# Second weight's sums alone through scratch, its plain blocks split in place, and the second phase's first loads on ScalarE's queue

## The reference, cut to what matters

```python
def reference(q, k, v, U, V, w_ch1, w_ch2, w_in, w_spatial, b_spatial, w_out):
    # windowed attention: batch 4, 8 heads, 576 tokens, head size 64, window 128
    x = attention(q, k, v)                      # (4, 576, 512)
    u = x + (x^T @ U @ V)^T                     # rank 32, over the tokens
    x = u + maximum(u @ w_ch1, 0) @ w_ch2       # w_ch1 512 x 2048, w_ch2 2048 x 512
    h = maximum(x @ w_in, 0); a, g = halves(h)
    g = layernorm(g); g = w_spatial @ g + b_spatial
    return (a * g) @ w_out                      # (4, 576, 512)
```

## Time and profile before

| what | us |
|---|---|
| median of 3 runs | 771.54 |
| lowest and highest | 770.56, 773.52 |
| the profiled execution, device time | 773.02 |
| its span, first to last instruction | 771.2 |
| PE busy in the span | 728.5 |
| VectorE busy | 454.9 |
| ScalarE busy | 339.0 |
| GpSimd busy | 180.3 |

### The profile page before, as it was taken

How to read it: one execution, slowest core, us unless ns; L and a number is a source line. 1 busy time by engine, 2 the same in 40 slices (tenths; PEclk the granted TensorE clock), 3 DMA queues, 4 the chain that set the end, 5 groups by cost and what they waited for, 6 DMA issues and landing times.

```text
span 771.2 us, 13217 instructions
## 1 busy us (share of the span) xinstructions
PE 728.5 (94%) x4688; PEld 671.2 (87%) x4688; DVE 454.9 (59%) x1036; ACT 339.0 (44%) x764; POOL 180.3 (23%) x187
## 2 busy tenths in 40 slices
PE   7999999988999978997679999999999999999998
PEld 5777777778999978997669999999999999998998
DVE  7778777888473247323495895795647417435431
ACT  5977777754352232222134444434343242342422
POOL 1868516410019999200000000000010000100100
PEclk9999999999999988998899999999999999999999
DMA  7689563155448997698975625754680010100101
GB/s 233 224 284 344 185 231 101 61 180 178 151 157 282 315 342 237 238 382 328 414 256 179 212 66 182 233 182 151 239 326 1 25 38 0 46 15 0 61 0 62
DMA packets 82514, 137.68 MB, mean 179 GB/s; under 512 B 5536, under 2 KB 57248, under 8 KB 81568
## 3 DMA queue, kind: packets, MB, share of 16 engines
q1 hardware_dynamic: 82464, 137.03, 51.2%
HBM read 80.06 MB, written 56.95 MB: 178 GB/s over the span
## 4 chain that ended last, share of the span: by engine, by line
PE 68%; DVE 12%; DMA 7%; POOL 5%; issue 4%; ACT 3%; SPq 1%; DVEq 0%; ACTq 0%; POOLq 0%
PE bank L1837 4%; PE bank L1839 4%; PE bank L1838 4%; PE bank L1679 3%; PE wide L1694 3%; PE bank L1876 3%; DMA r_scr<-late 3%; PE bank L1877 3%; PE bank L1878 3%; PE bank L1985 2%; PE bank L1987 2%; PE bank L1986 2%; PE bank L1804 2%; PE bank L1802 2%; PE bank L1803 2%
## 5 line engine op out<-in xcount | busy, mean ns | idle before, releaser
L1837 PE MATMUL bank<-xs,w1s 128*128 128x384 f32 x336 | 115.9, 345 | 9.9 <-DVE tok L1393 8.7
L1839 PE MATMUL bank<-xs,w1s 128*128 128x384 f32 x336 | 114.6, 341 | 0.0
L1838 PE MATMUL bank<-xs,w1s 128*128 128x384 f32 x336 | 114.6, 341 | 0.0
L868 POOL TENSOR_TENSOR vl<-vr,vh 128x512 fp32r<-128x512 f32 x8 | 11.3, 1407 | 401.5 <-ACT vh L1146 401.5
L1022 ACT ACTIVATE rk<-tok 128x768 fp32r<-128x768 f32 x72 | 60.6, 847 | 91.5 <-PE wide L1878 30.4
L1876 PE MATMUL bank<-rk,w2q 128*128 128x384 f32 x208 | 72.1, 347 | 18.4 <-DVE rk L1400 11.2
L1005 ACT ACTIVATE sums_u<-bank 128x384 f32<-128x384 f32 x72 | 35.4, 491 | 101.1 <-PE bank L1839 95.9
L881 ACT ACTIVATE sc<-sc,mn 128x256 f32<-128x256 f32 (+1 forms) x144 | 67.0, 468 | 21.3 <-DVE mn L1206 21.2
L1837 PEld LDWEIGHTS bank<-xs,w1s 128*128 128x128 f32 x336 | 65.0, 193 | 12.5 <-DVE tok L1393 9.9
L1877 PE MATMUL bank<-rk,w2q 128*128 128x384 f32 x208 | 70.5, 339 | 0.0
L1878 PE MATMUL bank<-rk,w2q 128*128 128x384 f32 x208 | 70.5, 339 | 0.0
(11 more groups left out here) (217 smaller groups left out, 1847.5 us busy)
## 6 DMA issues: line engine op xcount, KB each, us to landing
r_scr<-tok SPq DMA_DIRECT2D x19, 768.0 KB, 4.4
w2q<-w_scr SPq DMA_DIRECT2D x7, 2048.0 KB, 13.6
tok<-r_scr SPq DMA_DIRECT2D x18, 768.0 KB, 5.3
qkraw<-qk SPq DMA_DIRECT2D x32, 288.0 KB, 4.3
w1raw<-w SPq DMA_DIRECT2D x32, 256.0 KB, 4.6
wc_scr<-wprep SPq DMA_DIRECT2D x12, 512.0 KB, 4.1
w_scr<-tok SPq DMA_DIRECT2D x12, 512.0 KB, 3.6
u_scr<-tok SPq DMA_DIRECT2D x6, 768.0 KB, 4.9
```

Source lines behind the costliest of these rows:

```text
L1837: pe.matmul(o, wh, ah, start=(k == 0 and m in FRESH), stop=False, skip_group_check=True)
L1838: pe.matmul(o, wl, ah, start=False, stop=False, skip_group_check=True)
L1839: last = pe.matmul(o, wh, al, start=False, stop=(k == 1), skip_group_check=True)
```

## The change

Six things change together.

1. Only the four sums of the second weight go through `w2_scr`: GpSimd makes the sums of a unit and splits them in two pairs (`split_two`), each stored by one transfer; 8 instructions and two transfers (1 MB) a unit. A load waits for the sums to be formed (`w2_sum`) and not for a store to have landed; three buffers rotate (`w2_two`).
2. The plain blocks are loaded straight from `w_ch2`, 1 MB each, to the low half of `w2q[1]`, `w2q[2]` and `w2q[4]`, and GpSimd splits them there (`split_direct`); PE waits for that (`ready_in`).
3. Down's first loads (a, b, d, the plain blocks 1 and 2, and `w2q[6]`) are issued by ScalarE at steps 19 to 22 (`early`), ahead of `keep_p(s, 7)`; before, SyncE issued them. `LATE` is 18.
4. At step 23 ScalarE's first three `hi_r` stand ahead of `keep_p(23, 6)` and VectorE's first two `lo_r` ahead of `c11(23)`. `FIRST_T` puts two sums behind each of entries 5 to 12, `add_res(0, 11)` and `dc(0, 11)` move to entry 16, `add_res(0, 12)` to entry 17.
5. The last batch's `mix_up` uses two pairs of banks and runs up to two pairs ahead.
6. In the attention every `split_wc` comes a step later, the first loads for them too; the sums of unit 1 of the first weight are formed by GpSimd in step 2 (`w1_sum_1`) and not by VectorE at the start of up, and `c11(0)` moves behind `normalise(3, 3)`.

```diff
-W2_UNIT = {9: 0, 10: 1, 11: 2, 12: 3, 13: 4, 15: 5, 16: 6, 18: 7}
-LATE = 19
-WC_AFTER = {0: [0, 1], 1: [2, 3], 2: [4], 3: [5, 6], 4: [7, 8, 9], 5: [10, 11, 12], 6: [13], 7: [14, 15, 16]}
+W2_LOAD = {7: [0, 1], 9: [2], 10: [3], 11: [4], 12: [5], 15: [6], 16: [7]}
+W2_STORE = {9: 0, 10: 1, 11: 2, 12: 3, 13: 4, 14: 5, 17: 6, 18: 7}
+LATE = 18
+WC_AFTER = {1: [0, 1], 2: [2], 3: [3, 4], 4: [5, 6, 7], 5: [8, 9, 10], 6: [11], 7: [12, 13, 14], 8: [15, 16]}
+WC_LOAD = {p + 2: ms for p, ms in WC_AFTER.items()}
+WC_STORE = {p + 4: ms for p, ms in WC_AFTER.items()}
...
@@ SyncE
-            load_wc(0)
-            load_wc(1)
...
                 else:
-                    sp.wait_ge(w2_out_t, 4 * 16 * (kk - 1))
+                    sp.wait_ge(w2_sum, 4 * (kk - 1))
...
             def store_w2(kk):
...
+                for n in (2 * kk, 2 * kk + 1):
+                    q = S1 + 2 * (n % 2)
+                    sp.wait_ge(w2_low, n + 1)
+                    sp.dma_start(w2_scr[q:q + 2, :, kk].rearrange("q p h c -> p q (h c)"),
+                                 w2_two(n)).then_inc(w2_out[n % 3], 16)
...
+                if s in W2_STORE:
+                    store_w2(W2_STORE[s])
+                for kk in W2_LOAD.get(s, []):
+                    load_w2(kk)
...
@@ GpSimd
+            def split_two(n):
+
+                two = w2_two(n)
+                x, hi = two[:, :, QP:2 * QP], two[:, :, 0:QP].bitcast(F32R)
+                pool.tensor_copy(hi, x).then_inc(w2_hi, 1)
+                pool.wait_ge(w2_hi, n + 1)
+                pool.tensor_tensor(x.bitcast(F32R), x, hi, ALU.subtract).then_inc(w2_low, 1)
...
+                for n in (2 * kk, 2 * kk + 1):
+                    if n >= 3:
+                        pool.wait_ge(w2_out[n % 3], 16 * (n // 3))
...
+            def split_direct(m):
+
+                done = {1: 0, 2: 1, 4: 2}[m]
+                pool.wait_ge(weights_in[m], wc_loads(m) + 16)
+                for i in range(UNITS // 2):
+                    u = slice(2 * i, 2 * i + 2)
+                    x, hi = w2raw[m][:, u, 1], w2q[m][:, u, 0]
+                    pool.tensor_copy(hi, x).then_inc(w2_hi, 1)
+                    pool.wait_ge(w2_hi, 2 * UNITS + 4 * done + i + 1)
+                    pool.tensor_tensor(w2q[m][:, u, 1], x, hi, ALU.subtract).then_inc(ready_in, 1)
...
+                if p == 2:
+                    w1_sum_1()
...
@@ ScalarE
+            def early(s):
+
+                if s == LATE + 1:
+                    for i in range(3):
+                        act.wait_ge(w2_out[i], 16 * len(range(i, 2 * UNITS, 3)))
+                    act.wait_ge(xs_lo, 7 * G)
+                    for i in range(2):
+                        act.wait_ge(r_out[i], 16 * LATE // 2)
+                    early_raw("a")
+                elif s == 20:
+                    early_raw("b")
+                    early_direct(1)
+                elif s == 21:
+                    early_direct(2)
+                    early_raw("d")
+                elif s == 22:
+                    act.dma_start(w2q[6][:].bitcast(F32), w2_scr[WEIGHT[6]]).then_inc(weights_in[6], 16)
...
+                if LATE < s < NU - 1:
+                    early(s)
                 keep_p(s, 7)
...
@@ VectorE
-            w1_sum_of(1)
-            c11(0)
             normalise(B - 1, 3)
             w1_slow_of(1)
+            c11(0)
...
+                if s == NU - 1:
+                    lo_r(0)
+                    lo_r(1)
                 c11(s)
...
+                if n == ENTRY[(0, 7)]:
+                    add_res(0, 11)
+                    dc(0, 11)
+                elif n == ENTRY[(0, 7)] + 1:
+                    add_res(0, 12)
...
@@ TensorE
-                    if n >= 2:
-                        pe.wait_ge(u_kept, HEADROOM + b * 2 * KD + n - 1)
+                    if n >= 2 * ahead:
+                        pe.wait_ge(u_kept, HEADROOM + b * 2 * KD + n - 2 * ahead + 1)
...
-                    pe.wait_ge(weights_in[m], wc_loads(m) + 16)
+                    if m in (1, 2, 4):
+                        pe.wait_ge(ready_in, 4 * {1: 1, 2: 2, 4: 3}[m])
+                    else:
+                        pe.wait_ge(weights_in[m], wc_loads(m) + 16)
```

186 lines of the change are left out of this document (78 added, 108 removed).

## The result

| | before | after |
|---|---|---|
| time, median (lowest to highest), us | 772.0 (770.6 to 773.5) | 746.5 (745.9 to 747.4) |
| profiled execution, its span, us | 771.2 | 744.6 |
| granted TensorE clock, mean of the span | 0.982 | 0.993 |
| moved by DMA, MB | 137.7 | 128.2 |

The ratio is 0.9671, with a 95% interval of 0.9649 to 0.9692: 25.5 us faster, where 30.3 were forecast. 746.5 lies in the range on record (732 to 754) and 5.5 us above the forecast of 741.

What follows compares the result with a forecast made beforehand. Late up was taken as bound by the second weight's preparation (GpSimd 9.4 us a unit), with losses at the crossing and down's first sums. Terms sum to −30.3 us: median 771.5 to 741 (737 to 746, chance 0.5; eight in ten 732 to 754).

Steps and rivals of the forecast that it cites:

- Second weight beside up: Late up, 265 to 300 us: less GpSimd work, 8.7 us a unit, ends most of PE's 12.2 us loss; −9.2 us.
- change of group: Up, steps 15 and 16: VectorE's two-SBUF-tile operations slowed beside GpSimd's unit 6; some 3 us of loss remain.
- Crossing: Passage from up to down: two `lo_r` ahead of `c11(23)` let entry 0 follow (23,7); −7.1 us.
- First sums: Start of down, 371 to 410 us: later `add_res` ends VectorE's wait for `u_in`, VectorE's pace then bounds; −11.7 us.
- `mix_up` ahead: Near 190 us: PE's 2.36 us wait and the slow matmuls behind it go; −3.9 us.
- Attention: First `mix_down`: GpSimd's four extra sums make PE wait 2.0 us, outweighing 0.9 gained near 35 us; +1.1 us.
- Start of up: Beginning of up: PE's gains are waited out because ScalarE waits for unit 2's load, whose issue doesn't move; 0 us.
- ScalarE as issuer: Steps 19 to 22: three transfers at 0.77 us each make `keep_p(s, 7)` 0.2 to 0.3 late, twice; +0.5 us.
- One: Rival: nothing is left over, the group change and the attention's wait hide, terms at their good ends; 733 us, chance 0.12.
- Two: Rival: GpSimd late with the plain blocks, its splits slowing VectorE at down's first entries; about 752 us, chance 0.12.
- four: Rival: DMA engines full from step 19 on, crossing and first sums lose 4 us each; 749 us, chance 0.14.

Runs made afterwards that it cites:

- the run with lot 20 on SyncE: Changed kernel with only step 20's early transfers (block b and the first plain block) issued by SyncE, ScalarE keeping those of steps 19, 21 and 22: 749.9 us.

## Why the prediction was right, and where it was short

The gain is 25.5 us for 30.3, and the difference has names.

*Second weight beside up*, −8.3 for −9.2: right in size, and short in its cause. GpSimd's units started 8.6 us apart from 227.80 to 270.85 (8.7 in the forecast), no wait of PE stood in steps 9 to 14, and the last store landed as ScalarE asked for it, at 310.1. What is left at the change of group came with unit 5, not unit 6 (that waited 7.97 us for its load): 4.0, for 3 forecast, and 2.7 to 3.2 in the profiles that followed. Of it 1.2 stand there without GpSimd too, which the term put at nothing. But "Up late is bound by the preparation of the second weight. GpSimd needs 9.4 us a unit" named one of two limits that lay together. With GpSimd's work taken away, 6.8 of 12.3 us stayed, since the issue and the landing of six stores a unit took as long. The change cut both, to 6.7 us of work and two stores, and so the sum held.

*Crossing*, −7.3 for −7.1: entry 0 stands right behind (23,7). The forecast gave it all to the order; of it 4.4 are the order's, and 2.9 came with the rest of the change. The first plain block was split 4.3 us ahead of entry 0, not 8.

*First sums*, −12.1 for −11.7: first sum at +11.2 after (23,7) ended (+11.4 forecast), then 2.6 to 2.7 us an entry, VectorE without idle time, 3.7 us left of 4.0. The +32.5 of the forecast is eight periods of 2.63, as many as there are entries with two sums; the "seven periods and one `lo_r` more" of its words would give +30.7. The largest part was the wait that the forecast put first.

*`mix_up` ahead*, −4.3 for −3.9: no wait near 190 us; the slowed `mix_up` matmuls themselves came on top.

*Attention*, +2.6 for +1.1: this term failed in its size. The gap at 35 us went, and the wait of 2.0 came where and as long as forecast. It left out the slow clock behind that wait, 1.6 us in both profiles of the changed kernel, although it counted the slow matmuls behind other idle times. Half the profiled executions with the stall did not have it.

*Start of up*, 0 for 0: half of the reason was right. PE's waits of 1.22 for VectorE and of 0.29 and 0.75 for ScalarE went, and waits of 0.86 and 1.51 came, the latter for ScalarE, which stood 3.29 us before unit 2's load (1.27 before). So what VectorE was relieved of is waited out there, and moving that load was worth 3.1 us. But "whose issue doesn't move" was wrong: the load is issued behind two stores of the attention and moves with them, so what the attention gains or loses passes through.

*ScalarE as issuer*, +1.8 for +0.5, and 3.8 in the second profile: this step failed. "SyncE took 0.77 each" was read as the price of an issue. It was an issuing engine held up already: the first issue of a lot took 0.37 to 0.44, and those behind it 0.6 to 3.6 (the last of the lot in the run with lot 20 on SyncE). By the Trainium skill (DMA: Bandwidth & Descriptors, Issuing engines are not separate DMA queues) a second issuer only saves the sequencer's time, "which is usually small relative to the DMA itself". The first half agrees, with the loads on SyncE landing no later; the time saved here was SyncE's, which had it to spare, and the time spent ScalarE's, up to 5.5 us a lot.

The spans' difference, 26.6, falls 3.7 short of 30.3. The attention (1.5 more than forecast), ScalarE (1.3), the group change (0.9) and the program's start (0.8) make 4.5; the crossing, the sums and `mix_up` gave 1.0 more than forecast; 0.2 is rounding. Of the rivals, none came. One had the slices for it, which show no loss at the first group change; it is 1.2 us, too little for a slice to show. Two's contention exists, at 1 to 1.4 us beside unit 5, and not at down's first entries; four's full DMA engines exist too, at a share of 0.90 from 300 to 345 us, but the stores of up landed in 6.1 us, and the price was ScalarE's time to issue.

## What to carry to other kernels

Put a transfer on the queue of an engine that has nothing behind it. What an issue costs is not a constant: read it transfer by transfer where the DMA engines are as full as they will be, the first of a lot apart from those behind it, and take a long row for back pressure that will hold whichever engine issues. When one engine's work seems to set a pace, ask what the same pace would be with that work at zero: here issue and landing had the same length, and only a change that cut both could gain. And the price of a stall of 2 us is 2 us or 3.6, so count the second for the range.
